# Dense matrix products placed among attention's slots, value sums spread on chip, and the weights' first loads put behind three pairs of heads

## The reference, cut to what matters

```python
k_sum = k.reshape(B, H, 24, 32, D).max(axis=3)          # 24 block keys
v_sum = v.reshape(B, H, 24, 32, D).mean(axis=3)         # 24 block values
scores = [scale * q @ k.T masked to |i-j| < 16,  scale * q @ k_sum.T + log(32)]
a = exp(scores - max); a = a / (sum(a) + 1e-9)
x = a @ [v, v_sum]                                      # -> (B, S, 512)
h = relu(x @ w_in); u, v = h[..., :512], h[..., 512:]   # first mixer
v_n = (v - mean) / sqrt(var + 1e-6)
v_s = w_spatial @ v_n + b_spatial[:, None]
x = (u * v_s) @ w_out
h = relu(x @ w_in2)                                     # second mixer
c = conv of h over the tokens, 3 taps, conv_w
out = (h * sigmoid(c)) @ w_out2
```

## Time and profile before

| | |
|---|---|
| median of 3 runs | 374.37 us (374.15 to 376.27) |
| profiled execution, its own time | 374.59 us |
| its span | 372.6 us |
| TensorE busy | 350.8 us (94%) |
| VectorE, ScalarE, GpSimd busy | 223.2, 138.2, 73.0 us |
| mean granted TensorE clock | 0.975 of full |
| moved by DMA | 25.75 MB |

### The profile page before, as it was taken

One profiled execution on the slowest core, in us unless ns is written; L12 is line 12 of the kernel. 1 busy time (PEld: TensorE's weight loads), 2 busy tenths in 40 slices (PEclk: granted clock), 3 DMA queues, 4 the chain that ended last, 5 costly groups with the idle time before them and its releaser, 6 DMA issues.

```text
span 372.6 us, 6760 instructions
## 1 busy us (share of the span) xinstructions
PE 350.8 (94%) x2613; PEld 312.4 (84%) x2613; DVE 223.2 (60%) x572; ACT 138.2 (37%) x398; POOL 73.0 (20%) x87
## 2 busy tenths in 40 slices
PE   6598686989999999999999999999999999999996
PEld 6377565868889889999999988999999988889984
DVE  2759688596258367247644462368775557756662
ACT  3848577484255336341111122421222123122111
POOL 4314456364000000069100094000000000000000
PEclk9969899699999999999999999999999999999999
DMA  9999789864000201365100000000000003100004
GB/s 180 202 186 193 180 193 190 166 157 103 5 0 3 84 1 24 111 201 174 56 2 0 2 0 0 2 0 2 1 0 2 0 0 115 55 2 1 0 2 169
DMA packets 51604, 25.75 MB, mean 69 GB/s; under 512 B 44252, under 2 KB 46580, under 8 KB 51572
## 3 DMA queue, kind: packets, MB, share of 16 engines
q1 hardware_dynamic: 51572, 25.32, 29.1%
HBM read 20.98 MB, written 3.15 MB: 65 GB/s over the span
## 4 chain that ended last, share of the span: by engine, by line
PE 83%; DVE 5%; SPq 4%; issue 3%; ACT 2%; DMA 1%; ACTq 0%; DVEq 0%
PE bank L868 24%; PE bank L870 24%; PE bank L869 24%; PE bank L853 3%; ACT P L487 2%; PE bank L805 2%; PE bank L841 2%; DVE pT L628 2%; DVE SM L648 1%; PE bank L813 1%; SPq L277 1%; PE bank L909 1%; SPq L270 1%; PE bank L831 1%; DMA vw<-vs_s 1%
## 5 line engine op out<-in xcount | busy, mean ns | idle before, releaser
L870 PE MATMUL bank<-g_h,W_l 128*128 128x384 f32 x128 | 43.0, 336 | 0.0
L869 PE MATMUL bank<-g_l,W_h 128*128 128x384 f32 x128 | 42.9, 335 | 0.0
L868 PE MATMUL bank<-g_h,W_h 128*128 128x384 f32 x128 | 42.8, 334 | 0.0
L487 ACT ACTIVATE P<-SM,nmax 128x120 f32<-128x120 f32 x96 | 36.7, 384 | 12.6 <-DVE nmax L648 12.0
L870 PE MATMUL bank<-wo_h,hg_l 128*128 128x512 f32 x96 | 38.0, 396 | 0.0
L869 PE MATMUL bank<-wo_l,hg_h 128*128 128x512 f32 x96 | 38.0, 396 | 0.0
L868 PE MATMUL bank<-wo_h,hg_h 128*128 128x512 f32 x96 | 37.9, 395 | 0.0
L414 POOL TENSOR_TENSOR P<-P,rinv 128x480 f32<-128x480 f32 x24 | 23.7, 987 | 45.9 <-DVE rinv L635 45.9
L868 PE MATMUL bank<-wsT_h,vn_h 128*128 128x384 f32 x96 | 32.2, 335 | 0.0
L869 PE MATMUL bank<-wsT_l,vn_h 128*128 128x384 f32 x96 | 32.1, 334 | 0.0
L870 PE MATMUL bank<-wsT_h,vn_l 128*128 128x384 f32 x96 | 32.1, 334 | 0.0
(11 more groups left out here) (111 smaller groups left out, 803.5 us busy)
## 6 DMA issues: line engine op xcount, KB each, us to landing
stage<-in_moe_w_in SPq DMA_DIRECT2D x8, 512.0 KB, 4.3
vw<-in_v SPq DMA_DIRECT2D x16, 240.0 KB, 4.8
kn<-in_k SPq DMA_DIRECT2D x16, 192.0 KB, 3.6
qn<-in_q SPq DMA_DIRECT2D x16, 192.0 KB, 4.1
stage<-in_moe_w_out SPq DMA_DIRECT2D x6, 512.0 KB, 3.6
out<-obuf SPq DMA_DIRECT2D x12, 256.0 KB, 2.0
stage<-in_moe_w_spatial SPq DMA_DIRECT2D x6, 384.0 KB, 3.9
vw<-vs_s SPq DMA_DIRECT2D x32, 36.0 KB
```

Source lines behind the costliest of these rows:

```text
L487: a.activation(P[:, i % NP_, j, :], SM[:, i % 2, j, :], ACT.Exp, bias=nmax[:, c:c + 1], scale=-1.0, accum_out=rsum[:, c:c + 1]).then_inc(e ...
L868: t_.matmul(dst, lhs[0](c), rhs[0](c), start=first, stop=False)
L869: t_.matmul(dst, lhs[0](c), rhs[1](c), start=False, stop=False)
L870: ins = t_.matmul(dst, lhs[1](c), rhs[0](c), start=False, stop=last)
```

## The change

- **Scores.** `kw` becomes `kT`, one copy of the pair's keys with a pad at either end; a tile's local keys are a window of it. The block keys stay in `ks`. So each of the 8 score products of a group becomes two, one with 96 columns and one with 24. `fill_windows` goes.
- **Block values.** A second small product (`vp`, with the selector `psel`) puts the 24 sums on partitions 96 to 119; VectorE copies them to `vsum`, and GpSimd copies them into the 12 tiles of `vw` (`spread_sums`, 24 x 1536 elements). The 32 spreading DMAs go.
- **Banks.** Four banks (0 to 3) are a ring for units and dense units; scores keep two; pT and the values' output have one each in place of two.
- **Dense units among the slots.** wo in slots 3 and 4; one W unit in each of slots 7 to 13 and 15; the v units of batch 0 in slots 17 to 22; its u units in slots 23 to 27. Their order and that of the weights' items follow: wo, w2 (in half columns), wi, ws, wo2.
- **Splits.** GpSimd splits w2 and wi in 24 parts: from slot 1 on, two parts in a slot, one where i % 3 == 2. It now also splits v_n after attention.
- **Loads.** q of pairs 0 and 1 is issued by ScalarE. `stage` has 3 buffers. Order of SyncE: k 0, k 1, v 0, v 1, wo 0, k 2, q 2, wo 1, v 2, w2(0,0), and then the loop below.

```diff
-    NVB, NP_, NST = 3, 4, 4
+    NVB, NP_, NST = 3, 4, 3
...
+            units_at[GP * p] += [("k", p + 1, 0), ("k", p + 1, 1)] if more else []
+            units_at[GP * p] += [("vs", p, 0)]
+            units_at[GP * p + 1] += [("q", p + 1, 0), ("q", p + 1, 1)] if more else []
+            units_at[GP * p + 1] += [("vp", p, 0)]
+        fills_at[3] = [("wo", 0), ("wo", 1)]
+        fills_at[4] = [("wo", 2), ("wo", 3)]
+        for n, i in enumerate((7, 8, 9, 10, 11, 12, 13, 15)):
+            fills_at[i] = [("W", n % FC, n // FC)]
+        b0 = [("v", 0, m) for m in range(SC6)] + [("u", 0, f, n) for f in range(FC) for n in range(2)]
+        for n, i in enumerate((17, 18, 19, 20, 21, 22, 23, 24, 25, 25, 26, 26, 27, 27)):
+            fills_at[i].append(b0[n])
...
             load_k(0)
-            load_q(0)
             load_k(1)
-            load_q(1)
             sp.wait_ge(vpads, 2 * NVB)
             load_v(0)
             load_v(1)
-            sp.wait_ge(tr_done, tr_count(("k", 0, 1)))
+            load_item(0)
             load_k(2)
-            sp.wait_ge(tr_done, tr_count(("q", 0, 1)))
             load_q(2)
-            n = 0
+            load_item(1)
+            load_v(2)
+            load_item(2)
+            n = NST
             for p in range(NP):
-                for j in range(4):
-                    src = vs_s[32 * j:32 * j + QB, p % 2, :].unsqueeze(1).to_broadcast([QB, NT, 2 * D])
-                    sp.dma_start(vw[KW + QB * j:KW + QB * (j + 1), p % NVB, :, :], src).then_inc(vs_in[p % NVB], 16)
...
                 if p + 3 < NP:
                     load_k(p + 3)
-                if p < NP - 1:
+                if n < 9:
                     load_item(n)
                     n += 1
+                if p + 3 < NP:
+                    load_q(p + 3)
+                if 0 < p and p + 2 < NP:
+                    load_v(p + 2)
+                if p < 2 or 4 <= p:
+                    load_item(n)
+                    n += 1
...
+            def load_v(p):
+                if p >= NVB:
+                    sp.wait_ge(pv_done, GP * (p - NVB + 1))
...
+            def split_high(x, dh):
+                stage_wait(pool, x)
+                g.tensor_copy(dh, stage[:, item[x] % NST, :].rearrange("p (j m) -> p j m", j=2)).then_inc(split_hi, 1)
+            def split_low(x, e, dh, dl, done):
+                pool.wait_ge(split_hi, n_hi)
+                g.tensor_tensor(out=dl, in0=stage[:, item[x] % NST, e * 512:(e + 1) * 512], in1=dh.bitcast(fp32),
+                                op=ALU.subtract).then_inc(done, 1)
+            def spread_sums(p):
+                pool.wait_ge(vp_ready, p + 1)
+                src = vsum[KW:KA, p % 2, :].unsqueeze(1).to_broadcast([NB, NT, 2 * D])
+                g.tensor_copy(vw[KW:KA, p % NVB, :, :], src).then_inc(vb_ready, 1)
+            for i in range(1, SLOTS):
                 n = i - 1
+                if n < NG:
+                    pool.wait_ge(rinv_ready, n + 1)
+                    g.tensor_tensor(out=pi, in0=pi, in1=rinv[...], op=ALU.mult).then_inc(norm_done, 1)
+                if i % GP == 2 and i // GP < NP:
+                    spread_sums(i // GP)
+                for _ in range(1 if i % GP == 2 else 2):
+                    part = next(parts, None)
+                    if part is not None:
+                        split_part(part)
...
                 for h in range(2):
-                    at = h * KA
-                    for odd in range(2):
+                    for lo, n in ((0, KW), (KW, NB)):
+                        for odd in range(2):
...
+                                keys = kT[rows, p % 2, t * TQ:t * TQ + KW] if lo == 0 else ks[rows, p % 2, :]
...
+            for i in range(SLOTS):
                 if 3 <= i < NG + 3:
                     transpose_probs(i - 3)
                 if i < NG:
                     scores(i)
+                for u in units_at[i]:
+                    unit(u)
+                for u in fills_at[i]:
+                    dense(u)
+                if 4 <= i < NG + 4:
                     values(i - 4)
```

More of the change, by code:

```diff
@@ L174, in attention_mixer_program @@
+        s5_step, s5_done, o_act, o_dve = sem("s5_step"), sem("s5_done"), sem("o_act"), sem("o_dve")
         out_sem = [sem(f"out_done{i}") for i in range(4)]
-        units = []
-        units_of = {-1: [("k", 0, 0), ("k", 0, 1), ("q", 0, 0), ("q", 0, 1)]}
+        units_at = {i: [] for i in range(-1, SLOTS)}
+        units_at[-1] = [("k", 0, 0), ("k", 0, 1), ("q", 0, 0), ("q", 0, 1)]
         for p in range(NP):
             more = p + 1 < NP
[L182 to L185, removed]
@@ new lines, in attention_mixer_program, with bank_no @@
+        seq += [("v", 1, m) for m in range(SC6)]
+        seq += [wst.pop(0) for _ in range(4)]
+        for f in range(FC):
+            for n in range(2):
+                seq += [("u", 1, f, n), wst.pop(0)]
+        seq += [("cw",)]
+        S_AT = len(seq)
+        for b in range(B):
+            seq += [("s", b, f, n) for f in range(FC) for n in range(2)]
+        place = {u: n for n, u in enumerate(seq)}
+        def bank_no(n):
+            return n % 4 if n < ATT else (4 + n - ATT) % 8
@@ new lines, in attention_mixer_program @@
+        empties = {"k": tr_act, "q": tr_act, "vs": vs_ready, "vp": vp_ready, "wo": wol_ready, "W": Wl_ready,
+                   "v": v_relu, "u": u_ready, "ws": wsl_ready, "cw": cw_ready, "s": biased}
+        count, freed, before_it = {}, [], []
+        in_bank = {4: (max_ready, GT * NG), 5: (max_ready, GT * NG), 6: (pT_ready, NG), 7: (xl_ready, NG)}
+        for n, u in enumerate(seq):
+            e = empties[u[0]]
+            count[e] = count.get(e, 0) + 1
+            freed.append((e, count[e]))
+            before_it.append(in_bank.get(bank_no(n)))
+            in_bank[bank_no(n)] = freed[n]
@@ L235, in stage_free, with done_count, free_count @@
+        def done_count(u):
+            return place[u] + 1
+        def free_count(u):
+            return freed[place[u]][1]
+        items = [("wo", 0), ("wo", 1)] + [("w2", n, c) for n in range(2) for c in range(KC // 2)]
+        items += [("wi", c) for c in range(KC)] + [("ws", c) for c in range(SC6)] + [("wo2", c) for c in range(GC // 2)]
+        item = {x: n for n, x in enumerate(items)}
         def stage_free(eng, n):
@@ L259, in gate_out_wait, with load_heads @@
                 eng.wait_ge(s5_step, G + 1 - G // GC)
+        def load_heads(eng, dst, src, p, done):
+            b, h = p // PPB, 2 * (p % PPB)
+            for e in range(2):
+                eng.dma_start(dst[:, p % 2, :, e, :],
+                              src[b, h + e].rearrange("(c r) d -> r c d", r=128)).then_inc(done[p % 2], 16)
         block = ctx.enter_context(nc.Block())
@@ L398, in _ @@
             ins.then_inc(asel_ready, 1)
+            pool.wait_ge(asel_ready, 1)
+            in_turn(g.memset(psel[:, :, :], 0.0))
+            g.affine_select(out=psel[:, :, :], in_=psel[:, :, :], compare_op=ALU.not_equal, fill=1.0, base=0,
+                            pattern=[[-32, 4], [-1, QB]], channel_multiplier=1).then_inc(psel_ready, 1)
             n_hi = 0
-            def split(dh, dl, src, done):
+            def split_high(x, dh):
                 nonlocal n_hi
-                g.tensor_copy(dh, src).then_inc(split_hi, 1)
@@ new lines, in split_part @@
+            def split_part(n):
+                j, part = divmod(n, 3)
+                if j < KC:
+                    h, c = divmod(j, KC // 2)
+                    x, done = ("w2", h, c), w2_split
+                    cols = slice(h * 512, (h + 1) * 512)
+                    high = w2_h[:, 2 * c:2 * c + 2, cols]
+                    row = 2 * c + (part - 1)
+                    halves = (w2_h[:, row, cols], w2_l[:, row, cols]) if part else None
+                else:
+                    c = j - KC
+                    x, done = ("wi", c), wi_split
+                    high = wi_h[:, c, :].rearrange("p (j m) -> p j m", j=2)
+                    cols = slice((part - 1) * 512, part * 512)
+                    halves = (wi_h[:, c, cols], wi_l[:, c, cols]) if part else None
+                if part == 0:
+                    split_high(x, high)
+                else:
+                    split_low(x, part - 1, *halves, done)
@@ new lines, in _ @@
+            for t in range(B * SC6):
+                b, m = divmod(t, SC6)
+                pool.wait_ge(vn_ready, t + 1)
+                g.tensor_copy(vn_h[b][:, m, :], vraw[b][:, m, :]).then_inc(vnh_ready, 1)
+                pool.wait_ge(vnh_ready, t + 1)
+                g.tensor_tensor(out=vn_l[b][:, m, :], in0=vraw[b][:, m, :], in1=vn_h[b][:, m, :].bitcast(fp32),
+                                op=ALU.subtract).then_inc(vnl_ready, 1)
+            pool.wait_ge(gated, 2 * FC)
+            for c in range(GC // 2):
+                x = ("wo2", c)
+                stage_wait(pool, x)
+                rows = slice(2 * c, 2 * c + 2)
+                src = stage[:, item[x] % NST, :]
```

(48 more changed lines are left out.)

692 lines of the change are left out of this document (284 added, 408 removed).

## The result

The changed kernel takes 396.28 us (median of 4 runs, 394.98 to 397.80) against 374.50 for the one before on the same chips: ratio 1.057, 95% interval 1.051 to 1.063. The profiled execution took 394.98 us with a span of 393.3; I had forecast 393.0 and 391.0. (Two of the four runs had a span of 393.3, two of 395.8 and 396.0.)

What follows compares the result with a forecast made beforehand. TensorE was taken as the bound (83% of the chain), with about 32.5 us lost in attention's 99.33. Attention ending at 166.1 plus 224.9 behind it gave a span of 391.0; with 2.0 around it, 393.0 us, range 380 to 403.

Steps and rivals of the forecast that it cites:

- around the span: Time of the profiled execution outside its span, 2.0 us, added to the forecast span of 391.0.
- The two hold-ups: GpSimd waits for w2(0,0) and wi 3 ahead of norm(1) and norm(13); TensorE idles about 8 us and 9.2 us.
- The second rival: One hold-up is missing or the scores cost nothing: 382 to 386 us, two together 376; chance 0.25.
- The bytes: Loads up to w2(0,0): 5.65 MB in request order, q, k, v at about 182 GB/s, landing at 28.7 us.
- The slot: TensorE's pieces summed per attention slot, scores at 1.07 us: 5.99 with q and W, 5.13 without q.
- The part behind attention: Everything after attention: 273.3 us before, less 48.4 of units moved into the slots, leaves 224.9 us.
- ScalarE's loads of q: At the start, q on ScalarE's queue shares DMA with k of pair 0; first scores about 1 us later.
- the third rival: ScalarE's loads of q delay k of pair 0 about 1 us, hidden by slot 4's wait: no change to 393.
- 14 us of start: TensorE's loss up to slot 3, about 14 us, counted even if GpSimd isn't held up.
- 0.17 a unit: Extra cost of a W or v unit inside an attention slot: 2.73 us becomes 2.9.

Runs made afterwards that it cites:

- runs 1 to 3: Changed kernel with w2(0,0) requested ahead of pair 2 (391.05 us), with the item ahead of v from pair 4 on (387.67 us), with both (380.29 us).
- run 1: Changed kernel with w2(0,0) requested right behind wo 0, ahead of k, q and v of pair 2: 391.05 us, 1.046 to the kernel before.
- run 4: Changed kernel with the 8 score products of 24 columns in a group made twice: 400.56 us, 1.072 to the kernel before.
- run 6: Changed kernel with q of pairs 0 and 1 loaded by SyncE again, in the old place: 396.97 us, 1.060 to the kernel before.
- run 3: Changed kernel with w2(0,0) requested ahead of pair 2 and, from pair 4 on, the item ahead of v: 380.29 us, 1.016 to the kernel before.
- run 5: run 3 with the 14 v and u units of batch 0 in one block in the last slot: 393.80 us, 1.052 to the kernel before.
- run 10: run 5 with two banks for the values' output, three for the ring, and x_l behind the maxima: 394.59 us, 1.055 to the kernel before.

## Why the prediction was right, step by step

| step | forecast | measured |
|---|---|---|
| w2(0,0) there for GpSimd | 28.7 us | 28.50 |
| slot 4 starts | 32.2 | 31.87 |
| slot 7 starts | 43.6 | 44.80 |
| slot 15 ends | 94.4 | 95.7 |
| slot 16 starts | 103.6 | 104.31 |
| attention ends | 166.1 | 165.1 |
| the part behind it | 224.9 | 228.2 |
| around the span | 2.0 | 1.7 |

**The two hold-ups** are right in place, mechanism and size, and runs 1 to 3 show them as causes. The second rival gave 7 and 10.7 us for the absence of one, and 376 us without both; it was 5.2, 8.6 and 380.3. For the first the trace of run 1 shows why: TensorE met the next waits (2.7 and 1.77 us).

**The bytes.** The landing came out within 0.2 us, but partly by luck. The queues moved 215 GB/s up to 28.5 us, so the 5.65 MB of the sum had gone by about 26.6 us. w2(0,0) landed some 2 us behind that, when 6.1 MB had gone: 0.5 MB requested behind it, such as keys of pair 3 (issued at 23.83), went beside it. The price per byte was too high, and the order of landing too strict.

**The slot.** A slot with q and W came out at 5.97 for 5.99, but by two errors against each other. Scores were mis-sized: 64.14 to 64.83 is 0.69 us, not 1.07, so against the 0.57 of the earlier trace rows the split costs 0.12 a slot, some 3 us in all, not 12. (No run has the change without the split; run 4 gives 14 ns for a further record, which is in line.) The unit of q with vp was 1.13, not 0.86; transposes 0.59 and the W unit 2.94 were each 0.04 over. Without q the error shows: 69.52 to 74.35 is 4.83, forecast 5.13. Slot 7 took 7.48 for 5.99: its own waits for ScalarE's keys and VectorE's sums (0.25 and 0.95), not foreseen; slot 4 took 7.01 for 5.5. So slot 16 starts 0.7 late and attention still ends 1.0 early, again two errors against each other.

**The part behind attention** was 3.3 us over: the first v unit waits 0.9 for the last x_l, a further 1.7 stands before s (1.0) and gate_in (0.7), and 0.7 is not accounted for. The wait before s ends as VectorE finishes the low half of the last turned w_spatial (204.18 to 204.60; s starts at 204.71). In the kernel before, the wo transposes stood between the two: moving a unit away also uncovers what it hid. GpSimd's split of v_n and of wo2 is hidden, as costed.

**ScalarE's loads of q** cost 1.1 us at the start and nothing at the end (run 6), as the third rival said.

**What the prediction lacked** is why even a version without hold-ups loses. Run 3's span is 4.8 us longer than before (377.4 against 372.6): 3.3 of it in the part behind attention, as above, and 1.5 in attention. With the moved work priced as in the kernel before, run 3's attention ought to end at 99.33 + 48.4 = 147.7 if nothing were won; it ends at 149.2. Its stretches:

```profile
0.00:50.00 50.00, 37.69 (x558) 30.26 (x558) 27.03 (x120) 24.78 (x93) 29.26 (x45) 0.90 1.03 225
50.00:100.00 50.00, 48.90 (x726) 38.04 (x724) 29.21 (x125) 27.85 (x108) 29.03 (x26) 1.00 0.45 98
100.00:150.00 50.00, 49.26 (x567) 41.34 (x566) 22.82 (x99) 21.69 (x76) 9.83 (x9) 1.00 0.11 29
```

From 50 us on TensorE is full: filling works. But 12.3 us are idle before 50, and TensorE got new work: 0.12 in each of 24 slots, 0.4 in each q unit with its vp, 0.2 for each of 14 dense units between small products, an estimated 9 us in all from slot 10's rows. Idle time in attention fell only from 18.5 to 13.4 us. This is a sum of rows; no run takes the new work out. I took 14 us of start as given and 0.17 a unit, and saw none of it as the main term.

## What to carry to other kernels

When one in-order queue does both background work and a step of the critical chain, list for every wait in it what stands behind, and when the thing waited for can be requested at the earliest; two such waits cost 16 of the 22 us lost here, with TensorE and GpSimd both idle. Ask of each request also what it stands behind: wi 3 waited for a buffer that was not its own. Before filling an engine's gaps, add up what the fillers' banks, copies and switches cost; here the one bank for the values and the place of x_l cost next to nothing while slots are full and about 1 us in a bare one (run 5 against run 10), and the second bank, taken from the ring, cost as much again in the full ones.

## What the runs showed of the hardware that I had not expected

Products of 64 x 64 in four places of the array with 24 columns follow each other at 11 ns a record (8 from 64.35 to 64.44 us), with 96 columns at 26 (64.14 to 64.35); in run 4 further ones cost 14. The 120-column ones of the earlier trace rows take 36. The floor of about 25 ns from start to start that the prediction cited from the Trainium skill (TensorE: Matmul & The Clock Gate, "Wait — 56ns, not 53.3ns?") does not hold for them. The Trainium skill's same page, "Part 3: Packing small matmuls — row/col tiling", has products in different places of the array start some 4 ns apart. The trace agrees with that in so far as 11 is under 25; no run here shows 4.

GpSimd's copy of 24 partitions x 1536 elements took 1.46 us and its cast of 1024 columns 1.04, beside VectorE and ScalarE at work.
